# Expert layer's first product with the tokens' high and low parts as one moving operand of 512 columns

## What is computed

```python
# experts
logits = x @ w_gate; expert_idx = argmax(logits)
disp[e, counts[e]] = x[i]                     # the tokens of each expert
h = np.maximum(einsum('ecd,edf->ecf', disp, w1), 0.0)
y = einsum('ecf,efd->ecd', h, w2)
out[i] = gate_w[i] * y[expert_idx[i], pos[i]]
# feed-forward
h = x @ w_in
P = a[0] + a[1]*h + a[2]*h**2 + a[3]*h**3
Q = 1.0 + abs(b[0])*abs(h) + abs(b[1])*h**2
return (P / (Q + 1e-6)) @ w_out
```

## Time and profile before

| what | us |
|---|---|
| median of three runs | 547.32 |
| the profiled execution's own time | 546.42 |
| its span in the trace | 544.6 |
| PE busy | 535.7 (98%) |
| DVE busy | 405.6 (74%) |
| ACT busy | 320.1 (59%) |
| POOL (GpSimd) busy | 72.2 (13%) |

### The profile page before, as it was taken

How to read it: one execution, slowest core, us unless ns; L and a number is a source line. 1 busy time by engine, 2 the same in 40 slices (tenths; PEclk the granted TensorE clock), 3 DMA queues, 4 the chain that set the end, 5 groups by cost and what they waited for, 6 DMA issues and landing times.

```text
span 544.6 us, 8985 instructions
## 1 busy us (share of the span) xinstructions
PE 535.7 (98%) x3405; PEld 461.1 (85%) x3405; DVE 405.6 (74%) x738; ACT 320.1 (59%) x483; POOL 72.2 (13%) x71
## 2 busy tenths in 40 slices
PE   7999999999999999999999989999999999999997
PEld 5888889898998989899888878888888888888885
DVE  4667777654747456484889999998888888888885
ACT  3555634555636446465968785666666656665652
POOL 3333314601101010003010000003000000300000
PEclk9999999999999999999999999999999999999999
DMA  9999939959995574932160000001101000100002
GB/s 193 223 268 237 268 114 375 323 199 331 384 368 188 198 275 141 363 147 68 50 217 19 0 20 19 2 1 76 41 1 39 2 1 1 77 1 0 2 1 77
DMA packets 65039, 72.27 MB, mean 133 GB/s; under 512 B 41186, under 2 KB 41698, under 8 KB 64996
## 3 DMA queue, kind: packets, MB, share of 16 engines
q1 hardware_dynamic: 59268, 58.08, 34.3%
q0 software_dynamic: 3136, 9.46, 5.2%
q10 hardware_dynamic: 2592, 4.16, 2.1%
HBM read 59.09 MB, written 12.60 MB: 132 GB/s over the span
## 4 chain that ended last, share of the span: by engine, by line
PE 92%; DVE 3%; SPq 1%; ACT 1%; issue 1%; DMA 1%; DVEq 0%
PE bank L848 26%; PE bank L850 26%; PE bank L849 25%; PE bank L304 2%; PE bank L270 2%; PE bank L293 2%; SPq L1529 1%; PE bank L812 1%; PE bank L252 1%; PE bank L338 1%; PE bank L284 1%; PE bank L1135 1%; DMA kin<-in_k_dram 1%; PE bank L259 1%; PE bank L315 1%
## 5 line engine op out<-in xcount | busy, mean ns | idle before, releaser
L782 DVE TENSOR_TENSOR T<-raw,T 128x1024 fp32r<-128x1024 f32 x60 | 71.5, 1223 | 54.7 <-ACT T L776 53.7
L848 PE MATMUL bank<-x2H,T 128*128 128x512 f32 x192 | 75.5, 393 | 0.0
L848 PE MATMUL bank<-T,gL 128*128 128x512 f32 x192 | 74.8, 390 | 0.0
L850 PE MATMUL bank<-x2H,T 128*128 128x512 f32 x192 | 74.8, 390 | 0.0
L849 PE MATMUL bank<-x2L,T 128*128 128x512 f32 x192 | 74.8, 389 | 0.0
L850 PE MATMUL bank<-T,gH 128*128 128x512 f32 x192 | 74.8, 389 | 0.0
L849 PE MATMUL bank<-T,gH 128*128 128x512 f32 x192 | 74.7, 389 | 0.0
L848 PE MATMUL bank<-xH,T 128*128 128x256 f32 x256 | 72.5, 283 | 0.0
L849 PE MATMUL bank<-xL,T 128*128 128x256 f32 x256 | 72.4, 283 | 0.0
L850 PE MATMUL bank<-xH,T 128*128 128x256 f32 x256 | 72.4, 283 | 0.0
L1335 ACT ACTIVATE sq<-bank 128x512 f32<-128x512 f32 x48 | 28.5, 594 | 65.4 <-PE bank L850 65.2
(11 more groups left out here) (157 smaller groups left out, 1038.9 us busy)
## 6 DMA issues: line engine op xcount, KB each, us to landing
raw<-in_moe_w_dram SPq DMA_DIRECT2D x14, 2048.0 KB, 10.9
raw<-in_moe_w_dram SPq DMA_DIRECT2D x8, 512.0 KB, 4.6
w_out_raw<-in_moe_w_out_dram SPq DMA_DIRECT2D x4, 1024.0 KB, 16.6
ybuf<-ysb ACTq DMA_DIRECT2D x15, 256.0 KB, 5.9
qin<-in_q_dram SPq DMA_DIRECT2D x12, 256.0 KB, 5.1
kin<-in_k_dram SPq DMA_DIRECT2D x12, 256.0 KB, 5.6
vin<-in_v_dram SPq DMA_DIRECT2D x12, 256.0 KB, 5.6
xbuf<-xt SPq DMA_DIRECT2D x12, 256.0 KB, 4.1
```

Source lines behind the costliest of these rows:

```text
L782: e.tensor_tensor(W[w][:, 1, cols], raws[par][:, w, cols], W[w][:, 0, cols].bitcast(F32), ALU.subtract).then_inc(r.wL[w], 1)
L848: nc.tensor.matmul(out_, aL, bH, start=start, stop=False)
L850: return nc.tensor.matmul(out_, aH, bH, start=False, stop=stop)
```

## The change

The tokens' high and low parts lie in one tile, and one matmul with the high weights takes both (512 columns): its first half is high x high, its second half high x low. A second matmul adds low weights x high tokens to the second half. Each output tile now has a bank of its own, so a chunk takes two banks, 0 and 1 or 6 and 7. The two halves have to be added: ScalarE copies the second half to a new buffer `hs`, and takes hH as relu of the first half alone; VectorE adds the first half to `hs`, and makes hL from `hs` and hH. The `hL` count goes up twice per chunk. A chunk of `pe_up` waits for the sum of the chunk two before. `hs` lies where buffers of the routing lay, so the first copy waits for the routing's last use of these, and TensorE's second chunk for the routing's last reads of banks 6 and 7. VectorE's orders get the additions, and in the last expert the splits are placed anew. In the third layer the first group of transposes (s = 0) waits for `s_hf` 7, the second still for 8.

```diff
-        small_room = sb(early, "small_room", [P, TB * P * 2])
+        hs = [sb(early, f"hs{i}", [P, 2, NMAIN * P]) for i in range(2)]
-        xH = sb(early, "xH", [P, KD, NMAIN * P], F32R)
-        xL = sb(early, "xL", [P, KD, NMAIN * P], F32R)
+        xHL = sb(early, "xHL", [P, 2, KD, NMAIN * P], F32R)
+        xH, xL = xHL[:, 0, :, :], xHL[:, 1, :, :]
...
+        bank = [up_low[:, 0, :], up_low[:, 1, :]] + middle + [up_high[:, 0, :], up_high[:, 1, :]]
...
+        def two(out_, aH, aL, b, n, start, stop):
+            nc.tensor.matmul(out_[:, 0:2 * n], aH, b, start=start, stop=False)
+            return nc.tensor.matmul(out_[:, n:2 * n], aL, b[:, 0, :], start=False, stop=stop)
+        def sums(i, par, g):
+            return ((i * 2 + par) * HF + g) * 2 + 1
+        def lows(i, par, g):
+            return ((i * 2 + par) * HF + g) * 2 + 2
...
             for g in range(HF):
-                wait(e, r.hL, (i * 2 + par) * HF + (g - 1))
+                wait(e, r.hL, sums(i, par, g - 2))
+                if first and g == 1:
+                    e.wait_ge(s_index, 2)
+                    e.wait_ge(s_flag, 1)
...
-                        last = three(bank[g % 2][:, (f % 2) * n:(f % 2 + 1) * n], T0[:, 0, cols], T0[:, 1, cols],
-                                     xH[:, kk, 0:n], xL[:, kk, 0:n], kk == 0, kk == KD - 1)
+                        last = two(up_pair[g % 2][:, f % 2, :], T0[:, 0, cols], T0[:, 1, cols], xHL[:, :, kk, 0:n], n,
+                                   kk == 0, kk == KD - 1)
...
             e.wait_ge(r.mm1, (i * 2 + par) * HF + (g + 1))
-            e.activation(hH[:, 2 * g:2 * g + 2, 0:n], bank[g % 2][:, 0:2 * n].rearrange("p (a b) -> p a b", a=2),
-                         ACT.Relu).then_inc(r.hH, 1)
+            wait(e, r.hL, lows(i, par, g - 2))
+            if isinstance(i, int) and i + par + g == 0:
+                e.wait_ge(s_ex, 1)
+                e.wait_ge(s_gate, 8)
+            e.activation(hs[g % 2][:, :, 0:n], up_pair[g % 2][:, :, n:2 * n], ACT.Copy).then_inc(r.hH, 1)
+            e.activation(hH[:, 2 * g:2 * g + 2, 0:n], up_pair[g % 2][:, :, 0:n], ACT.Relu).then_inc(r.hH, 1)
+        def dve_sum(r, i, par, g):
+            e = nc.vector
+            n = r.nt * P
+            e.wait_ge(r.hH, lows(i, par, g))
+            e.tensor_tensor(hs[g % 2][:, :, 0:n], up_pair[g % 2][:, :, 0:n], hs[g % 2][:, :, 0:n],
+                            ALU.add).then_inc(r.hL, 1)
...
-            e.scalar_tensor_tensor(out=hL[:, 2 * g:2 * g + 2, 0:n],
-                                   in0=bank[g % 2][:, 0:2 * n].rearrange("p (a b) -> p a b", a=2), scalar=0.0,
+            e.wait_ge(r.hL, sums(i, par, g))
+            e.scalar_tensor_tensor(out=hL[:, 2 * g:2 * g + 2, 0:n], in0=hs[g % 2][:, :, 0:n], scalar=0.0,
...
+                dve_split(r, i, par, 1, 0)
                 for c in range(WC):
-                    dve_split(r, i, par, 1, c)
+                    dve_sum(r, i, par, c)
+                    if c + 1 < WC:
+                        dve_split(r, i, par, 1, c + 1)
                     dve_hL(r, i, par, c)
...
             if x2_no(bk, s) < 2:
-                e.wait_ge(s_hf, WIDE)
+                e.wait_ge(s_hf, WIDE - 1 + s)
...
         def dve_last_expert(r, i, par):
             for c in range(2):
                 dve_split(r, i, par, 1, c)
+            dve_sum(r, i, par, 0)
+            dve_split(r, i, par, 1, 2)
             dve_hL(r, i, par, 0)
-            for c in range(2, 4):
-                dve_split(r, i, par, 1, c)
+            dve_split(r, i, par, 1, 3)
+            dve_sum(r, i, par, 1)
             dve_hL(r, i, par, 1)
             dve_wout_ready(ready, 0)
+            dve_sum(r, i, par, 2)
             dve_hL(r, i, par, 2)
+            dve_sum(r, i, par, 3)
             dve_hL(r, i, par, 3)
```

More of the change, by code:

```diff
@@ L170, in build_program @@
         raws = [raw0, raw1]
-        bank = [ctx.enter_context(nc.psum_tensor(f"bank{i}", [P, 512], F32)) for i in range(8)]
+        up_low = ctx.enter_context(nc.psum_tensor("up_low", [P, 2, 512], F32))
+        middle = [ctx.enter_context(nc.psum_tensor(f"bank{i}", [P, 512], F32)) for i in range(2, 6)]
+        up_high = ctx.enter_context(nc.psum_tensor("up_high", [P, 2, 512], F32))
+        up_pair = [up_low, up_high]
+        bank = [up_low[:, 0, :], up_low[:, 1, :]] + middle + [up_high[:, 0, :], up_high[:, 1, :]]
         def cc(name):
@@ L741, in finish @@
                 for s, n in ((self.wL[0], WC * E), (self.wL[1], WC * E), (self.xL, self.nt * E),
-                             (self.hL, HF * E), (self.mm2, self.nt * E), (self.ys, self.nt * E),
+                             (self.hL, 2 * HF * E), (self.mm2, self.nt * E), (self.ys, self.nt * E),
                              (self.yst, 16 * self.nt * E)):
@@ L883, in dve_hL @@
             n = r.nt * P
-            e.wait_ge(r.hH, (i * 2 + par) * HF + (g + 1))
-            e.scalar_tensor_tensor(out=hL[:, 2 * g:2 * g + 2, 0:n],
-                                   in0=bank[g % 2][:, 0:2 * n].rearrange("p (a b) -> p a b", a=2), scalar=0.0,
+            e.wait_ge(r.hH, lows(i, par, g))
+            e.wait_ge(r.hL, sums(i, par, g))
+            e.scalar_tensor_tensor(out=hL[:, 2 * g:2 * g + 2, 0:n], in0=hs[g % 2][:, :, 0:n], scalar=0.0,
                                    in1=hH[:, 2 * g:2 * g + 2, 0:n].bitcast(F32), op0=ALU.max,
@@ L899, in pe_down @@
                     if s == 0 and kf % 2 == 0:
-                        e.wait_ge(r.hL, (i * 2 + par) * HF + (kf // 2 + 1))
+                        e.wait_ge(r.hL, lows(i, par, kf // 2))
                     toks, cols = slice(s * P, (s + 1) * P), slice(kf * DM, (kf + 1) * DM)
```

## The result

The changed kernel takes 545.24 us (median of seven runs, 545.02 to 545.49), the kernel before 546.50 in the same comparison (546.31 to 547.53): ratio 0.9971, interval 0.9959 to 0.9982. A later comparison of eleven against fifteen runs gave 0.9974 (0.9965 to 0.9983). It is faster, by 1.3 to 1.6 us. I had forecast 2.8 us less and 544.5 us. The range held the time; the size was twice too large. The seven runs of the kernel before lie in two groups, four at 546.3 to 546.5 us and three at 547.3 to 547.5, for a reason that no trace here shows; the changed kernel's lie in one. The forecast of 544.5 us started from a median in the upper group, and from the lower one it would have been 543.6, 1.6 us under the measured time. So that it came within 0.8 us is in part luck.

What follows compares the result with a forecast made beforehand. TensorE, busy 535.7 of 544.6 us, was taken as the bound. Experts -(7 x 0.42), waits +0.84 and +0.19, transposes -0.89 make -2.8 us, from 547.3 to 544.5; range from 543.0 less 0.2 for spread up to 546.8.

Steps and rivals of the forecast that it cites:

- Fewer matmuls: Experts' first product: three 256-column matmuls become one of 512 and one of 256, 0.3597 to 0.3465 us; 0.42 us saved per expert.
- What the fixed part is: TensorE's matmul steps: 0.013 us per matmul does not grow with columns, by the trace rows rather than the skill's 2.5 ns.
- One more instruction each on ScalarE and VectorE: Per chunk of the first product: 0.49 and 0.60 us more; waits before seven second products give back 0.84 us.
- The register wait: Four looped experts, between the matmuls' end and ScalarE's copy: 0.07 us each, bounded at 0.13.
- Buffers: TensorE's third and fourth chunks wait for the sum of the chunk two before; no cost.
- The last expert: Fourth chunk waits 0.61 us for VectorE's sum of chunk 1, so the second product starts 0.19 us later.
- The transposes' wait: Third layer: first transposes wait for one tile fewer; of 1.63 us, 0.89 stay, the rest is a new wait at tile 10.
- The wide matmul that is no cheaper: Rival, first product: a wide matmul costs as much as two narrow ones, 0.36 us a pair; 546.7 us, chance 0.11.
- The one in which the transposes' wait brings nothing: Rival, third layer: TensorE meets VectorE again at tile 10 with the full amount; 545.4 us, chance 0.14.
- The slower case: Rival, w2 chain before second products: delayed 0.52 us more in seven experts, plus register waits; 548.9 us, chance 0.08.

Runs made afterwards that it cites:

- the first attempt to mend the wait: Changed kernel, last expert: VectorE adds chunk 1 before splitting w2's last quarter, ScalarE scales gathered tiles before splitting w_in; 545.82 us in one run.

## Why the prediction was right and wrong, step by step

- **Fewer matmuls (forecast 0.42 us an expert).** This is the step that failed. The mechanism is right: a wide matmul is 0.013 us cheaper than two narrow ones, also with two runs, as the kernel of wide matmuls alone shows (0.2267 each). But I took each size's step from stretches of its own kind and added them, 0.3465. Alternating, they take 0.3528 in seven of the eight experts, and 0.0063 x 32 pairs is 0.20 us an expert: the seven first products gave 1.57 us and not 2.96. Of the 1.58 us that the forecast of the experts had too much this is 1.39; stalls 0.13 over their forecast and 0.22 in the last expert are the rest, less 0.17 that the second products gained. The value lies inside my bounds (0.3465 and 0.3597) near their middle; I took the end. A hint stood in the trace before: from 169.06 to 171.92, right behind the 128-column transposes of the earlier trace rows, twelve steps of the second product take 2.86 us, 0.14 more than at 0.2266, and I took this for an edge. (0.09 of it lies in the first step; the rest is spread over those behind.) That the sum of the two steps is reached in the first expert shows that it is no impossible value; which rhythm a stretch takes I can't forecast.
- **What the fixed part is.** The rows' 0.013 us held: 0.2267 us a wide matmul against twice 0.1199, and an expert's first product gained 0.22 us in spite of the alternation. The Trainium skill's page TensorE: Matmul & The Clock Gate, section Wait — 56ns, not 53.3ns?, gives a fixed 2.5 ns; by that figure the gain would be 0.08 us an expert, an estimate from that page, and the trace does not agree. The operands here are fp32r; whether that makes the difference no run here shows.
- **One more instruction each on ScalarE and VectorE.** Right in kind and order: 0.97 us of stalls against 0.84. That the totals are so near is partly luck: I had 0.15 us in each of four looped experts and 0.08 in three unrolled ones, and it was 0.20 or 0.21 in three looped ones, 0.36 in one, and nothing in the unrolled. The register wait cost ScalarE 0.09 us (I took 0.07 of at most 0.13), and a second 0.09 us lay in a place that I had not looked at, TensorE's own waits behind the blocking one. The unrolled experts had none: in the seventh TensorE is due 12.08 us after the expert's start, 0.20 later than forecast for its slower pairs, while VectorE's last quarter, which began behind three quarters of these pairs, ends at 11.97, 0.15 later than forecast.
- **Buffers.** Nothing there, as forecast: no chunk in the first seven experts waits for a sum.
- **The last expert.** Forecast a wait of 0.61 us, measured 0.38, and the second product 0.27 us late against 0.19. The wait is shorter because TensorE came later at the slower pairs and started 0.06 us after VectorE's end, not 0.14. I had named hL of chunk 3 as next in line; the first attempt to mend the wait ran into hL of chunk 2.
- **The transposes' wait.** Right: 0.89 us kept, the rest a new wait before tile 10, caused by ScalarE's w_out. Moving that work took the wait from 0.80 to 0.17 us, which shows the cause.
- **Rivals.** The wide matmul that is no cheaper came half true, though not from its two runs. The one in which the transposes' wait brings nothing is refuted by the kernel with the old wait. The slower case did not come; its chain was the right place but its delays were 0.2 us, not 0.5.

## What to carry to other kernels

Take the cost of a matmul from starts in the mix in which it will run: the sum of the steps of each size by itself was a lower end here, and grouping equal sizes gave about half of the difference back. Where an edit shortens the bound engine by a few per cent, list the slack of every chain that ends at it, because several were within 0.5 us here, and the stalls before the second products took back 0.97 of the 1.57 us that the first products gave. In a loop, put waits that are long met ahead of the one that blocks; behind it they cost 0.09 us on each of two engines here.

## What was not expected of the hardware

- Wide (512) and narrow (256) matmuls in turn take 0.3528 us a pair; alone their steps are 0.2266 and 0.1199. The wide ones have 0.010 us more, the narrow ones 0.003 less. Yet the same order also runs at 0.3466 us a pair over fourteen pairs of the first expert. Neither the two runs of the moving operand nor a single size alone makes the extra; why there are two rhythms is not settled.
- Waits against a register's value behind a blocking wait cost 0.09 us even when they are met: one on ScalarE, two together on TensorE.
- In some profiles of the changed kernel and its near relatives one looped expert shows 0.36 instead of 0.20 us of stall (the third in one, the fourth in two others, none in the rest). In the changed kernel's third expert VectorE ends at 145.07, as far into the expert as in the fourth, and TensorE starts at 145.45, 0.38 us later instead of 0.23; the trace gives nothing that it waited for in between. All three cases lie in the first of the loop's two passes. The cause is open.
